# Attention at the head of a three-stage kernel: probabilities as the stationary operand, v moved, rows normalised per partition and then transposed

## The chip, the cores and the metric

One core of a Trainium2 chip runs the whole program. The metric is the device time in microseconds (us) of one execution; the kernel before has a median of 1134.29 us over three runs (1134.02 to 1134.41).

## What is computed

Three stages follow each other: attention over 4 batches of 8 heads (576 rows, head size 64), a feed-forward layer, and a layer of 8 experts. The change touches the first stage alone.

```python
scores = scale * np.matmul(q, k.transpose(0, 1, 3, 2))
thresh = np.max(scores, axis=-1, keepdims=True) - tau
scores = np.where(scores >= thresh, scores, -1000000000.0)
scores = scores - np.max(scores, axis=-1, keepdims=True)
attn = np.exp(scores)
attn = attn / (np.sum(attn, axis=-1, keepdims=True) + 1e-09)
return np.matmul(attn, v).astype(np.float32)
...
x = np.ascontiguousarray(attn_out.transpose(0, 2, 1, 3)).reshape(B * S, H * D)
x = _moe_ref(x=x, **moe_kwargs)
return _moe2_ref(x=x, **moe2_kwargs)
```

## The kernel before

Attention works on 16 pairs of heads. The 576 rows of a pair fall into five chunks, c = 0 to 4: four of 128 rows for each of the two heads, and a last one in which the 64 remaining rows of both heads share the 128 partitions. A step is one chunk of one pair, so a pair takes five steps, and the order of the work on each engine is written out by hand as a loop over steps (TensorE L435, ScalarE L514, VectorE L607, GpSimd L295).

What is done to one chunk is spread over several steps. In step c the chunk's scores lie in PSUM (`scores`, L339, issued at the end of the step before; three products of high and low halves of q and k in a shortened float format, both heads side by side in the array as 64-row tiles). VectorE copies them out with a running maximum (`maximum`, L560), GpSimd makes the exponent's bias and the cut from it, ScalarE takes the exponential (L477), and a step later VectorE masks and sums (`mask`, L570). Two steps later TensorE transposes the probabilities in sets of three blocks (`transposed_probs`, L358) into two PSUM banks `t_ps` in turn, ScalarE copies each set out to `probs_T` (`evacuate`, L480), and three steps later `output_main` (L376) multiplies with v. There v is the stationary operand, 64 columns of it, and the probabilities move: the even head writes partitions 0 to 63 of `o_ps`, the odd head partitions 64 to 127, so that two 64-column tiles of the array work side by side; one product with `v_mix`, 128 columns wide, takes the block that both heads share. The result is already transposed, which is how the next stage wants it (`x_T`).

The row sums lie along partitions, the result's rows along columns. So `broadcast_rinv` (L395) spreads the reciprocals with eight small products into `m_ps`, ScalarE copies them to `rinv_bc` (`copy_rinv`, L497), and VectorE multiplies (`normalise_main`, L586). `output_tail` (L410) does the same for the last chunk, with `copy_rinv_tail` and `normalise_tail`.

`m_ps` is one PSUM bank shared by turns. It also takes the transposes of the next pair's k, q and ends (`transposed_k` L307, `transposed_q` L316, `transposed_ends` L326), which ScalarE copies as high halves (`k_hi`, `q_hi`, `ends_hi`) and VectorE turns into low halves (`k_lo`, `q_lo`, `ends_lo`). A turn ends when the low half is done.

Two waits set the rhythm between TensorE and VectorE: scores of a step wait until both maxima of the step before are done (their two PSUM tiles are reused, L343), and the transposes of a chunk wait for its masks (L361). In a set's wait on `evac_done` (L363) the transposes wait for the set two before it to be copied out.

## Time and profile before

| | us |
|---|---|
| median of three runs | 1134.29 |
| lowest, highest | 1134.02, 1134.41 |
| the profiled execution: its time | 1132.23 |
| the profiled execution: its span, first to last instruction | 1130.5 |
| TensorE matmul busy, in all | 1046.8 (93% of the span) |
| weight loads busy | 925.7 (82%) |
| VectorE, ScalarE, GpSimd busy | 678.1, 556.1, 495.1 |
| mean granted TensorE clock | 0.977 |

Attention ends and the feed-forward layer's first product starts at 335.21 us of the span. In the trace an operand pair is written output<-moving,stationary or the other way round; which one is stationary is told by the weight load (PEld) rows. A product of 32-bit floats shows as two MATMUL records, each with its own weight load, called two passes here; a transpose shows as one. The form 128\*64 is a tile of 128 rows by 64 columns of the array, and what follows is the moving operand. Durations of matmuls overlap, so costs are read from one start to the next. c = 0 to 4 names the step; "two heads" marks scores of steps 0 to 3, "ends" those of step 4.

### The profile page before, as it was taken

The page shows a single profiled execution, that of the slowest core. Times are in us where ns is not written, and L with a number is a line of the kernel's source. Part 1 is how long each engine was busy: PE and PEld are TensorE (multiplying, and loading weights), DVE is VectorE, ACT ScalarE, POOL GpSimd, SP SyncE. Part 2 cuts the span into 40 slices and gives each one's busy share as a digit, 9 for nine tenths or more (in the row PEclk, how much of TensorE's full clock was granted, in tenths as well). Part 3 has the DMA queues.
Part 4 walks back from the last instruction along what each step waited for, and adds up shares of the span by engine and source line. Part 5 has one row for each costly group of instructions (what it writes and reads, how often), then busy time and mean ns, then how long its engine had stood idle before and what let it go on. Part 6 is the DMA issues. An engine that isn't in the chain of part 4 may idle for free. (4 is left out here: it accounts for less than half of the span.)

```text
span 1130.5 us, 22630 instructions
## 1 busy us (share of the span) xinstructions
PE 1046.8 (93%) x8153; PEld 925.7 (82%) x8153; DVE 678.1 (60%) x1336; ACT 556.1 (49%) x854; POOL 495.1 (44%) x734
## 2 busy tenths in 40 slices
PE   7999999999989999999899999997489999999995
PEld 5778787877769999999899989996377777777774
DVE  5887887878756534334334433433667777777773
ACT  4777777778753211211121112111367777777773
POOL 4777777777740000000000000000548888888973
PEclk9999999999999999999999999998599999999999
DMA  4323232232112100000000000002492573411100
GB/s 105 79 63 80 50 86 55 67 76 64 37 49 76 29 20 1 25 1 19 2 24 1 19 2 24 1 19 71 151 394 94 179 254 106 178 39 37 38 27 22
DMA packets 76314, 75.40 MB, mean 67 GB/s; under 512 B 48815, under 2 KB 54959, under 8 KB 76210
## 3 DMA queue, kind: packets, MB, share of 16 engines
q1 hardware_dynamic: 72690, 63.49, 18.4%
q0 software_dynamic: 3520, 10.49, 2.7%
q8 instruction: 69, 1.13, 0.4%
q14 instruction: 35, 0.29, 0.1%
HBM read 64.52 MB, written 10.49 MB: 66 GB/s over the span
## 5 line engine op out<-in xcount | busy, mean ns | idle before, releaser
L820 ACT ACTIVATE r_buf<-h_ps 128x288 f32<-128x288 f32 x128 | 52.6, 411 | 347.3 <-PE h_ps L777 347.3
L884 DVE TENSOR_TENSOR r_buf<-r_buf 128x288 f32<-128x288 f32 x128 | 58.7, 458 | 243.5 <-ACT r_buf L820 243.5
L1169 POOL MEMSET ones<- 128x128 bf16 x1 | 0.2, 209 | 453.0 <-POOLq L637 453.0
L1097 DVE TENSOR_TENSOR w_lo<-w_experts,w_hi 128x2048 fp32r<-128x2048 f32 x66 | 163.4, 2501 | 32.1 <-ACT w_hi L1336 32.1
L1336 ACT ACTIVATE w_hi<-w_experts 128x2048 fp32r x88 | 163.4, 1909 | 32.1 <-issue 14.0
L777 PE MATMUL h_ps<-x_hi,w_in_hi 128*128 128x288 f32 x512 | 154.4, 302 | 6.1 <-DVE x_lo L878 3.5
L777 PE MATMUL h_ps<-x_hi,w_in_lo 128*128 128x288 f32 x512 | 151.9, 297 | 3.1 <-issue 3.1
L777 PE MATMUL h_ps<-x_lo,w_in_hi 128*128 128x288 f32 x512 | 152.4, 298 | 0.0
L796 PE MATMUL y_ps<-g_hi,w_out_hi 128*128 128x288 f32 x512 | 151.4, 296 | 0.3 <-DVE g_lo L890 0.3
L796 PE MATMUL y_ps<-g_hi,w_out_lo 128*128 128x288 f32 x512 | 151.1, 295 | 0.0
L796 PE MATMUL y_ps<-g_lo,w_out_hi 128*128 128x288 f32 x512 | 151.0, 295 | 0.0
L477 ACT ACTIVATE e_sb<-s_sb,stats,live 128x576 f32<-128x576 f32 x144 | 124.4, 865 | 22.8 <-POOL stats L263 21.4
L576 DVE SCALAR_TENSOR_TENSOR probs<-s_sb,stats,e_sb 128x576 f32<-128x576 f32 x144 | 115.7, 835 | 1.5 <-POOL stats L276 1.4
L567 DVE TENSOR_SCALAR_CACHE_REDUCE s_sb<-s_ps 128x576 f32<-128x576 f32 x144 | 103.7, 754 | 19.0 <-PE s_ps L353 17.9
L777 PEld LDWEIGHTS h_ps<-x_hi,w_in_hi 128*128 128x128 f32 x512 | 97.2, 190 | 10.0 <-issue 9.9
L263 POOL TENSOR_SCALAR stats<-stats,minus_live 128x1 f32<-128x1 f32 x144 | 76.0, 528 | 61.3 <-DVE s_sb L567 60.8
L1097 POOL TENSOR_TENSOR w_lo<-w_experts,w_hi 128x2048 fp32r<-128x2048 f32 x22 | 101.9, 4633 | 2.0 <-ACT w_hi L1336 1.7
L495 ACT ACTIVATE probs_T<-t_ps 128x384 f32<-128x384 f32 x192 | 86.5, 485 | 32.6 <-PE t_ps L368 27.9
L777 PEld LDWEIGHTS h_ps<-x_hi,w_in_lo 128*128 128x128 f32 x512 | 97.6, 191 | 0.0
L777 PEld LDWEIGHTS h_ps<-x_lo,w_in_hi 128*128 128x128 f32 x512 | 97.4, 190 | 0.0
L796 PEld LDWEIGHTS y_ps<-g_hi,w_out_hi 128*128 128x128 f32 x512 | 96.6, 189 | 0.6 <-DVE g_lo L890 0.6
L796 PEld LDWEIGHTS y_ps<-g_hi,w_out_lo 128*128 128x128 f32 x512 | 96.6, 189 | 0.0
(196 smaller groups left out, 2407.0 us busy)
## 6 DMA issues: line engine op xcount, KB each, us to landing
w_experts<-in_moe_w_dram SPq DMA_DIRECT2D x16, 2048.0 KB, 13.9
k_raw<-in_k_dram SPq DMA_DIRECT2D x32, 128.0 KB, 3.1
q_raw<-in_q_dram SPq DMA_DIRECT2D x32, 128.0 KB, 3.0
w_raw<-in_moe_w_in_dram SPq DMA_DIRECT2D x16, 256.0 KB, 3.2
v_nat<-in_v_dram SPq DMA_DIRECT2D x16, 256.0 KB, 2.6
y_T<-in_moe_w_out_dram SPq DMA_DIRECT2D x16, 256.0 KB, 2.7
y_rows<-y_row SPq DMA_DIRECT2D x16, 256.0 KB, 2.2
v_odd<-in_v_dram SPq DMA_DIRECT2D x16, 64.0 KB, 2.3
```

The source lines that it names most:

```text
L263: V.tensor_scalar(stat(BIAS, step, h), stat(MAX, step, h), minus_live[:], None, ALU.mult).then_inc(bias_ready, 1)
L477: nc.scalar.activation(e_sb[step % 2][h][:], s_sb[step % 2][h][:], ACT.Exp, bias=stat(BIAS, step, h), scale=live[:]).then_inc(exp_done, 1)
L495: nc.scalar.activation(out, src[:], ACT.Copy).then_inc(evac_done, 1)
L567: V.tensor_scalar(halves(s_sb[step % 2][h][:]), s_ps[n % 2][:, :, 0:HALF], 1.0, None, ALU.mult, ALU.max, accum_out=stat(MAX, step, h)).the ...
L576: V.scalar_tensor_tensor(probs_of(c, h), s_sb[step % 2][h][:], stat(CUT, step, h), e_sb[step % 2][h][:], ALU.is_ge, ALU.mult, accum_out=su ...
L777: last = pe.matmul(h_ps[f % 2][:, 0:HALF], w, x[hf][:, kc, :], start=(kc == 0 and m == 0), stop=(kc == KC - 1 and m == 2))
L796: last = pe.matmul(y_ps[d][:, 0:HALF], w, g[f % 2][:], start=(f == 0 and m == 0), stop=(f == FC - 1 and m == 2))
L820: nc.scalar.activation(r_buf[f % 2][:], h_ps[f % 2][:, 0:HALF], ACT.Relu).then_inc(relu_done, 1)
L884: nc.vector.tensor_tensor(r[:], r[:], r[:], ALU.mult).then_inc(g_ops, 1)
L1097: alu.tensor_tensor(group_of(w_lo, g), raw_group(buf, g), group_of(w_hi, g).bitcast(F32), ALU.subtract).then_inc(done, 1)
L1169: nc.gpsimd.memset(ones[:], 1.0).then_inc(pool_set, 1)
L1336: nc.scalar.activation(group_of(w_hi, g), raw_group(buf, g), ACT.Copy).then_inc(hi_done, 1)
```

## The change

Seven things change, all in attention.

- `output_main`: the transposed probabilities become the stationary operand (128 columns), v moves (64 columns, and 128 for `v_mix`). The result has rows on partitions and is not transposed.
- `normalise_main` multiplies by the reciprocal per partition into a new tile `x_nat`; `broadcast_rinv`, `copy_rinv` and `copy_rinv_tail` are gone.
- `transposed_x` transposes `x_nat` with four transposes into `m_ps`, in step 3 of the next pair; ScalarE copies it to `x_T` (`copy_x`).
- `output_tail` moves from step 2 to step 3, waits for `copy_x`, and has five products 128 columns wide instead of twelve of 64; `normalise_tail` becomes two operations on 64 x 64 at the end of step 4; `transposed_x_tail` brings the two halves into place with one product against `ident2`, followed by a scores product in TensorE's order; ScalarE copies it in the step after.
- Ends are padded from 64 to 128 rows or columns with zeros (six more memsets in the set-up).
- Low halves move later on VectorE: `k_lo` from the end of step 0 to behind the maxima of step 1, `q_lo` from step 1 to the end of step 2, `ends_lo` from step 3 to behind the maximum of step 4. `q_hi` moves to step 2 and `ends_hi` to step 4 on ScalarE.
- `transposed_x` waits for `q_lo` of the next pair, `transposed_q` for `k_lo`.

```diff
@@ TensorE
             def output_main(i, c):
...
+                pt, even, odd = probs_T[m % 2], slice(c * P, c * P + D), slice(c * P + D, (c + 1) * P)
+                pe.matmul(o_ps[:, c * P:(c + 1) * P], pt[:, LAST, :], v_mix[b][:], start=True, stop=False,
+                          skip_group_check=True)
                 for kc in range(LAST):
-                    pe.matmul(o_ps[0:D, cols], v_nat[b][:, 0, kc, :], pt[:, kc, :],
-                              start=(c == 0 and kc == 0), stop=False, skip_group_check=True)
-                    pe.matmul(o_ps[D:P, cols], v_odd[b][:, kc, :], pt[:, LAST + 1 + kc, :],
-                              start=(c == 0 and kc == 0), stop=False, skip_group_check=True)
-                pe.matmul(o_ps[:, cols], v_mix[b][:], pt[:, LAST, :], start=False, stop=(c == LAST - 1),
-                          skip_group_check=True).then_inc(pv_done, 1)
+                    pe.matmul(o_ps[:, even], pt[:, kc, :], v_nat[b][:, 0, kc, :], start=False, stop=(kc == LAST - 1),
+                              skip_group_check=True)
+                for kc in range(LAST):
+                    last = pe.matmul(o_ps[:, odd], pt[:, LAST + 1 + kc, :], v_odd[b][:, kc, :], start=False,
+                                     stop=(kc == LAST - 1), skip_group_check=True)
+                last.then_inc(pv_done, 1)
...
             def output_tail(i):
                 b = i % 2
                 pe.wait_ge(evac_done, set_no(i, LAST, 1) + 1)
-                pe.wait_ge(rbc_done, i + 1)
+                pe.wait_ge(x_main_done, i + 1)
+                for kc in range(QC):
+                    last = pe.matmul(m_ps[:, TAIL_OUT:TAIL_OUT + P], tail_T[:, kc, :], v_nat[b][:, :, kc, :],
+                                     start=(kc == 0), stop=(kc == LAST))
+                last.then_inc(tail_set, 1)
+
+            def transposed_x(i):
+                pe.wait_ge(norm_done, i + 1)
                 if i + 2 < PAIRS:
                     pe.wait_ge(qlo_done, i + 3)
...
+                for c in range(LAST):
+                    last = pe.transpose(m_ps[:, c * P:(c + 1) * P], x_nat[:, c, :], ident[:])
+                last.then_inc(x_main_set, 1)
+
+            def transposed_x_tail(i):
+                pe.wait_ge(norm_tail_done, 2 * (i + 1))
...
+                pe.matmul(m_ps[:, TAIL_X:TAIL_X + TAIL], x_nat[:, LAST, :], ident2[:], start=True,
+                          stop=True).then_inc(x_tail_set, 1)
...
@@ VectorE
             def normalise_main(i):
                 dve.wait_ge(pv_done, LAST * (i + 1))
-                dve.wait_ge(rbc_done, i + 1)
-                V.tensor_tensor(x_T[:, i, 0:MAIN], o_ps[:], rinv_bc[:, 0:MAIN], ALU.mult).then_inc(x_main_done, 1)
+                dve.wait_ge(rinv_ready, i + 1)
+                if i >= 1:
+                    dve.wait_ge(x_main_set, i)
+                each = rinv[:, 0:2 * LAST].rearrange("p (n a) -> p n a", a=1).broadcast_to([P, 2 * LAST, D])
+                V.tensor_tensor(x_nat[:, 0:LAST, :].rearrange("p c (h d) -> p (c h) d", h=2),
+                                o_ps[:].rearrange("p (n d) -> p n d", d=D), each, ALU.mult).then_inc(norm_done, 1)
...
+                for h in range(2):
+                    rows = slice(h * TAIL, (h + 1) * TAIL)
+                    V.tensor_scalar(x_nat[rows, LAST, h * D:(h + 1) * D],
+                                    m_ps[rows, TAIL_OUT + h * D:TAIL_OUT + (h + 1) * D], rinv[rows, CHUNKS - 1:CHUNKS],
+                                    None, ALU.mult).then_inc(norm_tail_done, 1)
```

How the instructions stand now is shown for the two engines that wait for each other. First TensorE, from the transposes in step 2 on (L368 and L375 are the probabilities' transposes, L353 and L360 the scores). Before:

```order
L368 MATMUL t_ps<-ident,probs 128x128 x9
L417 MATMUL m_ps<-ident,rinv 64x64 x2
L423 MATMUL m_ps<-tail_T,v_nat 64x64 x10
L353 MATMUL s_ps<-kT_hi,qT_hi 128x288 x4
L353 MATMUL s_ps<-kT_lo,qT_hi 128x288 x4
L353 MATMUL s_ps<-kT_hi,qT_lo 128x288 x4
L368 MATMUL t_ps<-ident,probs 128x128 x6
```

The same place in the changed kernel, on through step 3:

```order
L375 MATMUL t_ps<-ident,probs 128x128 x9
L360 MATMUL s_ps<-kT_hi,qT_hi 128x288 x4
L360 MATMUL s_ps<-kT_lo,qT_hi 128x288 x4
L360 MATMUL s_ps<-kT_hi,qT_lo 128x288 x4
L375 MATMUL t_ps<-ident,probs 128x128 x6
L420 MATMUL m_ps<-ident,x_nat 128x128 x4
L394 MATMUL o_ps<-v_mix,probs_T 128x128
L397 MATMUL o_ps<-v_nat,probs_T 128x64 x4
L400 MATMUL o_ps<-v_odd,probs_T 128x64 x4
L375 MATMUL t_ps<-ident,probs 128x128 x3
L409 MATMUL m_ps<-v_nat,tail_T 128x128 x5
L343 MATMUL m_ps<-ident,q_raw 128x128
```

The tail's products have left step 2, which now holds nine transposes and the scores; they stand in step 3, together with the four new transposes of x.

Then VectorE, from the end of step 0 to step 3 (L567 and L570 are maxima, L576 and L579 masks, L543 and L546 `k_lo`, L548 and L551 `q_lo`, L589 and L595 `normalise_main`). Before:

```order
L543 TENSOR_TENSOR kT_lo<-m_ps,kT_hi 128x512
L584 RECIPROCAL rinv<-sums_eps 128x9
L567 TENSOR_SCALAR s_sb,stats<-s_ps 128x576 x2
L576 SCALAR_TENSOR_TENSOR probs,sums<-s_sb,stats,e_sb 128x576 x2
L548 SCALAR_TENSOR_TENSOR qT_lo<-m_ps,qT_hi 128x512
L567 TENSOR_SCALAR s_sb,stats<-s_ps 128x576 x2
L589 TENSOR_TENSOR x_T<-o_ps,rinv_bc 128x512
L576 SCALAR_TENSOR_TENSOR probs,sums<-s_sb,stats,e_sb 128x576 x2
L567 TENSOR_SCALAR s_sb,stats<-s_ps 128x576 x2
```

In the changed kernel:

```order
L570 TENSOR_SCALAR s_sb,stats<-s_ps 128x576 x2
L546 TENSOR_TENSOR kT_lo<-m_ps,kT_hi 128x512
L579 SCALAR_TENSOR_TENSOR probs,sums<-s_sb,stats,e_sb 128x576 x2
L587 RECIPROCAL rinv<-sums_eps 128x9
L570 TENSOR_SCALAR s_sb,stats<-s_ps 128x576 x2
L595 TENSOR_TENSOR x_nat<-o_ps,rinv 128x512
L579 SCALAR_TENSOR_TENSOR probs,sums<-s_sb,stats,e_sb 128x576 x2
L551 SCALAR_TENSOR_TENSOR qT_lo<-m_ps,qT_hi 128x512
L570 TENSOR_SCALAR s_sb,stats<-s_ps 128x576 x2
```

`q_lo` now stands behind the normalisation and both masks of step 2, where before it stood ahead of the maxima of that step.

## Rows read from the trace of the kernel before

**Rows 1.** The page, part 1: busy time by engine.

```profile
PE 1046.8 (93%) x8153; PEld 925.7 (82%) x8153; DVE 678.1 (60%) x1336; ACT 556.1 (49%) x854; POOL 495.1 (44%) x734
```

**Rows 2.** Stretches, one pair: us; busy PE, PEld, DVE, ACT, POOL; clock; DMA.

```profile
202.23:221.94 19.71, 19.24 (x219) 15.69 (x218) 15.93 (x44) 15.26 (x30) 14.68 (x39) 1.00 0.29 67
```

**Rows 3.** Timeline of TensorE, one pair: start, duration, then the instructions.

```profile
202.23 0.27 PE L336 MATMUL m_ps<-ident,q_raw 128*128 128x128 f32 x1
...
202.63 0.53 PE L353 MATMUL s_ps<-kT_hi,qT_hi 128*128 128x288 f32 x2
...
204.28 0.32 PE L388 MATMUL o_ps<-probs_T,v_nat 128*64 128x128 f32 x1
...
205.63 0.49 PE L368 MATMUL t_ps<-ident,probs 128*128 128x128 f32 x3
206.05 0.53 PE L353 MATMUL s_ps<-kT_hi,qT_hi 64*128 64x288 f32 x4
...
210.04 0.54 PE L353 MATMUL s_ps<-kT_hi,qT_hi 64*128 64x288 f32 x4
...
211.23 1.09 PE L405 MATMUL m_ps<-ident,rinv 128*64 128x128 f32 x16
212.26 0.66 PE L371 MATMUL t_ps<-ident,probs 128*128 128x128 f32 x4
...
215.82 0.88 PE L368 MATMUL t_ps<-ident,probs 128*128 128x128 f32 x6
217.04 0.52 PE L368 MATMUL t_ps<-ident,probs 128*128 128x128 f32 x3 [0.34 <-ACT probs_T L495]
217.49 0.33 PE L417 MATMUL m_ps<-ident,rinv 128*64 128x64 f32 x4
217.65 0.90 PE L423 MATMUL m_ps<-tail_T,v_nat 128*64 128x64 f32 x20
218.48 0.53 PE L353 MATMUL s_ps<-kT_hi,qT_hi 64*128 64x288 f32 x4
...
219.46 0.87 PE L368 MATMUL t_ps<-ident,probs 128*128 128x128 f32 x6
```

**Rows 4.** Timelines of TensorE and its weight loads, second stage: 128 stationary columns.

```profile
401.38 0.60 PE L749 MATMUL row_ps<-ident,y_T 128*128 128x128 f32 x4
401.81 0.96 PE L751 MATMUL logit_ps<-gates,y_T 128*128 128x16 f32 x8
401.70 0.97 PEld L751 LDWEIGHTS logit_ps<-gates,y_T 128*128 128x128 f32 x8
402.59 0.19 PEld L777 LDWEIGHTS h_ps<-x_hi,w_in_hi 128*128 128x128 f32 x1
```

**Rows 5.** Timeline of VectorE in the same pair.

```profile
215.57 0.69 DVE L548 SCALAR_TENSOR_TENSOR qT_lo<-m_ps,qT_hi 128x512 fp32r<-128x512 f32 x1 [1.51 <-ACT qT_hi L466]
...
217.53 0.69 DVE L589 TENSOR_TENSOR x_T<-o_ps,rinv_bc 128x512 f32<-128x512 f32 x1
218.13 0.81 DVE L576 SCALAR_TENSOR_TENSOR probs<-s_sb,stats,e_sb 128x576 f32<-128x576 f32 x1
...
218.86 0.82 DVE L576 SCALAR_TENSOR_TENSOR probs<-s_sb,stats,e_sb 128x576 f32<-128x576 f32 x1
...
219.60 0.76 DVE L567 TENSOR_SCALAR_CACHE_REDUCE s_sb<-s_ps 128x576 f32<-128x576 f32 x1
...
220.28 0.76 DVE L567 TENSOR_SCALAR_CACHE_REDUCE s_sb<-s_ps 128x576 f32<-128x576 f32 x1
```

**Rows 6.** Groups by line, 50 to 320 us: busy, mean ns, idle before.

```profile
L501 ACT ACTIVATE rinv_bc<-m_ps 128x512 f32<-128x512 f32 x14 | 8.4, 597 | 14.1 <-PE m_ps L405 14.1
...
L593 DVE TENSOR_TENSOR x_T<-m_ps,rinv_bc 128x64 f32<-128x64 f32 x14 | 3.1, 221 | 0.0
```

**Rows 7.** Timeline of TensorE at the end of attention.

```profile
330.20 0.49 PE L392 MATMUL o_ps<-probs_T,v_mix 128*128 128x128 f32 x2
...
335.21 0.58 PE L777 MATMUL h_ps<-x_hi,w_in_hi 128*128 128x288 f32 x1 [3.53 <-DVE x_lo L878]
```

More of the change, by code:

```diff
@@ L134, in attention @@
         rinv = sb("rinv", [P, CHUNKS])
-        rinv_bc = sb("rinv_bc", [P, S])
+        x_nat = sb("x_nat", [P, QC, P])
+        ident2 = sb("ident2", [P, TAIL])
         tau_col = sb("tau_col", [P, 1])
@@ L178, in attention @@
         WPIECE = WPART // LAST
+        SETUP = 14
+        Q_END, K_END, TAIL_OUT, TAIL_X = 0, P, 2 * P, 3 * P
         def qk_bank(i, kind):
@@ L372, in transposed_probs @@
                 else:
-                    last = pe.transpose(out[0:TAIL, 0:P], probs[c][:, MAIN:S], ident[:])
+                    last = pe.transpose(out[:, 0:P], probs[c][:, S - P:S], ident[:])
                 last.then_inc(probs_set, 1)
@@ L392, in output_main @@
-                pe.matmul(o_ps[:, cols], v_mix[b][:], pt[:, LAST, :], start=False, stop=(c == LAST - 1),
-                          skip_group_check=True).then_inc(pv_done, 1)
-            def broadcast_rinv(i):
-                pe.wait_ge(rinv_ready, i + 1)
-                if i + 2 < PAIRS:
-                    pe.wait_ge(klo_done, i + 3)
-                else:
-                    pe.wait_ge(elo_done, 2 * PAIRS)
-                    pe.wait_ge(x_tail_done, i)
-                    pe.wait_ge(rbc_tail_done, i)
-                for c in range(LAST):
-                    for par in range(2):
-                        last = pe.matmul(m_ps[D * par:D * (par + 1), c * P:(c + 1) * P],
-                                         rinv[:, 2 * c + par:2 * c + par + 1].broadcast_to([P, D]), ident[:],
-                                         start=True, stop=True)
-                last.then_inc(rinv_set, 1)
+                    pe.matmul(o_ps[:, even], pt[:, kc, :], v_nat[b][:, 0, kc, :], start=False, stop=(kc == LAST - 1),
+                              skip_group_check=True)
@@ L434, in _ @@
             scores(0, 0)
-            for step in range(STEPS * PAIRS + 3):
+            for step in range(STEPS * PAIRS + STEPS):
                 i, c = divmod(step, STEPS)
                 made, used = divmod(step - 2, STEPS), divmod(step - 3, STEPS)
-                if c == 1 and i >= 1:
-                    broadcast_rinv(i - 1)
                 if 0 <= made[0] < PAIRS:
@@ L444, in _ @@
                     transposed_k(i + 1)
-                if 0 <= used[0] and used[1] < LAST:
+                if c == 3 and i >= 1:
+                    transposed_x(i - 1)
+                if 0 <= used[0] < PAIRS and used[1] < LAST:
                     output_main(*used)
@@ L450, in _ @@
                     transposed_q(i + 1)
-                if 0 <= used[0] and used[1] == LAST:
-                    output_tail(used[0])
+                if c == 3 and i >= 1:
+                    output_tail(i - 1)
                 if c == 3 and i + 1 < PAIRS:
                     transposed_ends(i + 1)
+                if c == 4 and i >= 1:
+                    transposed_x_tail(i - 1)
                 if step + 1 < STEPS * PAIRS:
@@ L513, in _ @@
             act.wait_ge(live_set, 2)
-            for step in range(STEPS * PAIRS + 3):
+            for step in range(STEPS * PAIRS + STEPS + 1):
                 i, c = divmod(step, STEPS)
                 made = divmod(step - 2, STEPS)
-                if c == 1 and i >= 1:
-                    copy_rinv(i - 1)
+                if c == 0 and i >= 2:
+                    copy_x_tail(i - 2)
+                if c == 4 and i + 1 < PAIRS:
+                    ends_hi(i + 1)
                 if 0 <= made[0] < PAIRS:
@@ L525, in _ @@
                     k_hi(i + 1)
+                if c == 2 and i + 1 < PAIRS:
+                    q_hi(i + 1)
+                if c == 3 and 1 <= i <= PAIRS:
+                    copy_x(i - 1)
                 if 0 <= made[0] < PAIRS and sets_in(made[1]) == 3:
                     evacuate(*made, 2)
[L528 to L533 removed]
                 if i < PAIRS and len(heads_in(c)) == 2:
@@ L606, in _ @@
             ends_lo(0)
-            for step in range(STEPS * PAIRS + 4):
+            for step in range(STEPS * PAIRS + STEPS):
                 i, c = divmod(step, STEPS)
@@ L612, in _ @@
                         maximum(i, c, h)
+                if c == 1 and i + 1 < PAIRS:
+                    k_lo(i + 1)
                 if c == 2 and i >= 1:
                     normalise_main(i - 1)
-                if c == 3 and i >= 1:
-                    normalise_tail(i - 1)
+                if c == 4 and i + 1 < PAIRS:
+                    ends_lo(i + 1)
                 if 0 <= before[0] < PAIRS:
@@ L619, in _ @@
                         mask(*before, h)
-                if c == 0 and i + 1 < PAIRS:
-                    k_lo(i + 1)
-                if c == 0 and i >= 1:
+                if c == 1 and i >= 1:
                     reciprocal(i - 1)
-                if c == 1 and i + 1 < PAIRS:
+                if c == 2 and i + 1 < PAIRS:
                     q_lo(i + 1)
-                if c == 3 and i + 1 < PAIRS:
-                    ends_lo(i + 1)
+                if c == 4 and i >= 1:
+                    normalise_tail(i - 1)
 EARLY = HALF // P
```

97 lines of the change are left out of this document (45 added, 52 removed).

## The prediction

> **What bounds the kernel now.** I began with the busy shares: TensorE is busy for 93% of the span, no other engine for more than 60% [rows 1]. Then I cut out one pair of attention: from one transpose of the ends to the same one of the next pair is 19.71 us, with TensorE busy for 19.24, VectorE 15.93, ScalarE 15.26, at full clock (1.00, the 2.4 GHz level) [rows 2]. The two pairs after it read the same. So attention is TensorE's queue, read start to start. It stands still in two places: nine transposes in step 2 take from 215.82 to 217.04 before the last three begin, because both banks wait for ScalarE's copy, where six in a row would take 0.71; that is 0.51. And from scores to the broadcast of the reciprocals is 1.19 (210.04 to 211.23), from scores to transposes 0.98 (218.48 to 219.46), so 0.21 there. Waits are 0.7 a pair, work is 19.0 [rows 3]. Whatever TensorE gets more of is paid in full.
>
> **Prices.** Four transposes take 0.43 (401.38 to 401.81), so 0.108 each [rows 4]. Three transposes and a change of the array's tile shape take 0.42 (205.63 to 206.05): a change costs 0.10 [rows 3]. The form that decides is a float product with 128 stationary columns and few moving: its eight passes have eight weight loads, from 401.70 to the next load at 402.59, 0.111 each [rows 4]. These passes move only 16 columns, so moving less doesn't help: the load sets the pace. The other bound is what a pass costs if its 64 moving columns decide: the tail's 20 passes in side-by-side pairs need 0.83 (217.65 to 218.48); less two changes of shape that is 0.063 a pair [rows 3]. I take 0.111, since its row has the same stationary width; the tail's has half of it.
>
> **The multiplication with v.** Before: 204.28 to 205.63 is 1.35, plus the change into 64-column tiles 0.10, so 1.45 [rows 3]. Now nine products of two passes, 18 x 0.111 = 2.00, and no change of shape. That is +0.55 a chunk, +2.2 a pair. The eight pairs of passes that ran side by side at 0.109 (0.87 together) become 16 in a row (1.78), and only two changes of shape come off. The Trainium skill, TensorEngine Tiling (Array Packing), When to Use Tiling, recommends the opposite swap where the moving side has 64 columns or fewer: make it stationary and use two column tiles, up to twice as fast. By that rule 0.87 becomes 1.74, and the trace agrees with it. Its Key Properties say that a change of tiling mode drains the engine, which speaks for the change; the trace prices that at 0.10.
>
> **The rest of TensorE's work, per pair** [rows 3].
> - Broadcasts go: 211.23 to 212.26, -1.03.
> - The tail: 217.49 to 218.48 is 0.99; now 5 x 2 passes at 0.111 = 1.11; +0.12.
> - Four transposes of x: +0.43. Joining the tail's halves: 2 passes, +0.22.
> - Ends: 202.23 to 202.63 is 0.40; now two full transposes without a change of shape, 0.22; -0.18.
> - The last probability block, 128 columns for 64: same slot, 0.
> Sum: 2.2 - 1.03 + 0.12 + 0.43 + 0.22 - 0.18 = +1.8 a pair; work becomes 20.8.
>
> **The waits.** Time 0 is here the start of the scores of chunk 2, which TensorE issues at the end of step 1. VectorE's first maximum starts 1.12 later (218.48 to 219.60), each takes 0.68 (219.60 to 220.28), the normalisation 0.60 (217.53 to 218.13), a mask 0.73 (218.13 to 218.86), and a result is seen by TensorE at its full duration plus about 0.06, a mask's and a maximum's with 0.08 more for the accumulator [rows 5]. In the changed order VectorE does: maxima at 1.12 and 1.80, normalisation at 2.49, masks at 3.09 and 3.83, `q_lo` at 4.57 (done 5.32), maxima of step 3 at 5.18 and 5.86, masks to 8.0.
> - Step 2 on TensorE: transposes at 0.98, the last three at 2.20 behind ScalarE as before, scores at 2.65. The maxima allow 2.63. Without the tail nothing else fills this step. Wait 0.51.
> - Step 3: transposes could begin at 3.63; the first mask is seen at 3.93 (wait 0.30), the second at 4.67 (0.36), `q_lo` at 5.32 (0.30). Then transposes of x, v (2.00), three transposes: 8.12. The tail needs `copy_x` on ScalarE, which stands behind an exponential fed by the maximum at 5.18; I put its end at 7.8, 0.60 long [rows 6], so just in time. Tail and ends: scores of chunk 4 at 9.45.
> - Step 4: VectorE has the maximum at 10.54, `ends_lo`, two masks, then the two halves of the tail's normalisation, each at most the 0.22 of today's [rows 6], and done near 13.5. TensorE would be there at 13.3. Wait 0.15, scores at 13.8. Behind `transposed_x_tail` stand the next pair's first scores, so this wait would be everybody's.
> - Step 0 takes 4.55; step 1 4.12, and `k_lo` is seen 3.24 after its scores where TensorE needs it at 3.59: no wait.
> Waits are 1.67 and the period 13.8 + 4.55 + 4.12 = 22.47 against 19.71: +2.77. VectorE (about 16 busy) and ScalarE keep up over the whole pair; it is their order in steps 2 and 3 that binds. GpSimd is at 14.68 of 19.71 [rows 2] and keeps pace in each step but the shortest, where it has slack till the masks.
>
> **The ends of the stage.** Fourteen full pairs: +38.8. The first has two chunks only, +0.9. The last one waits more for its masks in any case and loses k, q and ends in both kernels, +2.2. Then a chain that was short before: from the last product with v (330.20) to the next stage's first (335.21) is 5.0 [rows 7]. New in line are the normalisation 0.69, transposes 0.43 and copy 0.60, and the tail, its normalisation, joining and copy follow one after another: about 3.6 of work for 1.4, and four more hand-overs of 0.2 (a transpose runs 0.27, its slot is 0.11 [rows 3]); +3.2. More memsets and `ident2` at the start hide behind the first loads; without that cover they would be 1.5. Loads of v start a step later and still have most of a pair. Sum: 38.8 + 0.9 + 2.2 + 3.2 = **+45**. The profiled execution was 1132.23, its span 1130.5; it becomes 1177. The median is 2.1 above it, so 1179.
>
> **Rivals.**
> - *The order absorbs its waits.* VectorE and ScalarE run ahead in the long steps, waits stay at 0.7. For it: `q_lo` has 1.51 of idle time ahead of it today [rows 5]. Against it: the maxima of chunk 2 can't start before its scores. +1.8 x 16 + 3 = +32, less for the ends of the stage, 1165.
> - *More waits than I traced.* `copy_x` comes late behind the exponential, or the tail's normalisation does: each delay passes through to the scores. One more us a pair gives +61, 1195.
> - *Loads hide in part.* A pass half-way between the bounds, 0.087: v 1.57 a chunk, but then `copy_x` holds step 3 and VectorE step 4; traced again the period is 21.1, +1.4 x 15 + 3 = +24, 1158. The Trainium skill, TensorE: Matmul & The Clock Gate, Back-to-back issue gap, gives about 81 ns a matmul for load-and-multiply streams of 128; the estimate by it is 1156. Rows 4 speak against it here.
> - *Faster.* A pass costs what its 64 moving columns cost, 0.063. The 84 passes a pair save 4.0, work is 16.8. With waits as today the period is 17.5, or -2.2 x 15 + 3 = -30, 1104; it decides from a pass below 0.090 (the 1.8 of more work over 84). Against it: the 16-column passes, and by my trace VectorE's order would still hold the period at 20.4 (1147).
> - *No change.* It would need a pass near 0.090 and waits that don't grow; nothing in the rows gives both.
> A clock that falls is no rival: the single waits are under 0.6 and clock stayed at 1.00 over such waits [rows 2].
>
> **How the numbers follow.** Forecast 0.58; waits absorbed 0.15; more waits 0.15; loads hidden in part 0.06; faster 0.03; no change 0.02; more than all of these 0.01. The range takes in the forecast, the absorbed waits and half of the third, and a pass at 0.108 or 0.114 (4 us): 1163 to 1193, leaving out 0.06 + 0.07 + 0.06, about 0.2. A measurement of this kernel can tell 0.2%, 2.3 us. Faster 0.03, same 0.02, slower 0.95.
>
> **What would show it.** The period of a pair near 22.5. The passes of the product with v 0.11 apart, a chunk 2.0. TensorE idle in step 2 before the last three transposes, and in step 3 ahead of both sets and ahead of the transposes of x, released by VectorE's masks and `q_lo`; almost no wait at the tail. No records at 64-column tiles in attention. The second stage's first product near 380. I am wrong if passes of `output_main` are closer than 0.09, if the period is under 21.4 or over 23.5, or if waits stand mostly elsewhere, for instance at `transposed_x_tail`.

## The result and the profile after

The changed kernel takes 1184.81 us (median of four runs, 1183.98 to 1186.32) against 1134.15 for the kernel before (four runs, 1132.51 to 1134.41): a ratio of 1.0451, with a 95% interval of 1.0433 to 1.0469. That is 50.7 us more. The profiled execution of the changed kernel took 1186.32 with a span of 1184.6, so the spans differ by 54.1.

The busy shares, part 1 of the page of the changed kernel, answer to [rows 1]:

```profile
PE 1085.9 (92%) x7769; PEld 986.3 (83%) x7769; DVE 679.3 (57%) x1359; ACT 555.9 (47%) x854; POOL 489.2 (41%) x734
```

TensorE has fewer records than before (7769 for 8153) and is busy for 39 us longer; the others do what they did. One pair, in the view of stretches, answers to [rows 2]:

```profile
207.25:229.82 22.57, 21.45 (x196) 19.26 (x195) 15.92 (x44) 15.18 (x30) 14.52 (x39) 1.00 0.24 60
```

The period is 22.57 for 19.71. The 54.1 us of span fall into four pieces, read at the last scores, at the first product of the second stage and at the first of the third:

| | before | after | difference |
|---|---|---|---|
| last scores of attention | 319.96 | 363.92 | +44.0 |
| from there to the second stage's first product | 15.25 | 19.05 | +3.8 |
| second stage (code unchanged) | 453.6 | 458.8 | +5.2 |
| third stage (code unchanged) | 341.7 | 342.8 | +1.1 |

The rows that they are read at, besides the two first products of the second stage (335.21 and 382.97): before,

```profile
319.96 0.51 PE L353 MATMUL s_ps<-kT_hi,qT_hi 128*128 128x288 f32 x2
...
788.82 0.31 PE L1220 MATMUL he_ps<-ohb,earlier 128*128 128x160 bf16 x1 [4.78 <-DVE ohb L1397]
```

and changed,

```profile
363.92 0.51 PE L360 MATMUL s_ps<-kT_hi,qT_hi 128*128 128x288 f32 x2
...
841.76 0.32 PE L1238 MATMUL he_ps<-ohb,earlier 128*128 128x160 bf16 x1 [4.78 <-DVE ohb L1415]
```

The timeline of TensorE in that pair answers to [rows 3] (start, duration, instructions):

```profile
208.93 0.39 PE L394 MATMUL o_ps<-v_mix,probs_T 128*128 128x128 f32 x2
209.15 1.00 PE L397 MATMUL o_ps<-v_nat,probs_T 128*128 128x64 f32 x8
209.99 1.06 PE L400 MATMUL o_ps<-v_odd,probs_T 128*128 128x64 f32 x8
210.89 0.50 PE L375 MATMUL t_ps<-ident,probs 128*128 128x128 f32 x3
211.62 0.43 PE L428 MATMUL m_ps<-ident,x_nat 128*128 128x64 f32 x2 [0.23 <-DVE x_nat L604]
211.98 0.53 PE L360 MATMUL s_ps<-kT_hi,qT_hi 64*128 64x288 f32 x4
...
220.58 0.53 PE L360 MATMUL s_ps<-kT_hi,qT_hi 64*128 64x288 f32 x4
...
222.79 0.52 PE L375 MATMUL t_ps<-ident,probs 128*128 128x128 f32 x3 [0.34 <-ACT probs_T L502]
223.24 0.54 PE L360 MATMUL s_ps<-kT_hi,qT_hi 64*128 64x288 f32 x4
...
224.51 0.55 PE L375 MATMUL t_ps<-ident,probs 128*128 128x128 f32 x3 [0.20 <-DVE probs L579]
225.25 0.55 PE L375 MATMUL t_ps<-ident,probs 128*128 128x128 f32 x3 [0.19 <-DVE probs L579]
225.95 0.63 PE L420 MATMUL m_ps<-ident,x_nat 128*128 128x128 f32 x4
...
228.70 1.28 PE L409 MATMUL m_ps<-v_nat,tail_T 128*128 128x128 f32 x10
229.82 0.27 PE L343 MATMUL m_ps<-ident,q_raw 128*128 128x128 f32 x1
```

Two things are to be seen. Eight passes of L397 take 0.84 (209.15 to 209.99), so 0.105 each, and a whole chunk takes 2.0 (208.93 to 210.89). And between 223.24 and 225.95 both sets of transposes stand behind VectorE's masks. VectorE's own timeline shows why (it answers to [rows 5]):

```profile
221.68 0.76 DVE L570 TENSOR_SCALAR_CACHE_REDUCE s_sb<-s_ps 128x576 f32<-128x576 f32 x1 [0.44 <-PE s_ps L360]
...
223.03 0.69 DVE L595 TENSOR_TENSOR x_nat<-o_ps,rinv 128x512 f32<-128x512 f32 x1
223.64 0.81 DVE L579 SCALAR_TENSOR_TENSOR probs<-s_sb,stats,e_sb 128x576 f32<-128x576 f32 x1
...
224.37 0.81 DVE L579 SCALAR_TENSOR_TENSOR probs<-s_sb,stats,e_sb 128x576 f32<-128x576 f32 x1
...
225.11 0.69 DVE L551 SCALAR_TENSOR_TENSOR qT_lo<-m_ps,qT_hi 128x512 fp32r<-128x512 f32 x1
...
231.04 0.76 DVE L570 TENSOR_SCALAR_CACHE_REDUCE s_sb<-s_ps 128x576 f32<-128x576 f32 x1 [2.41 <-PE s_ps L360]
```

The maximum of chunk 2 can't start before its scores (220.58), and from 221.68 to 225.71 VectorE has no gap; the transposes of x wait for `q_lo` at the end of it. Once the masks of step 3 are done, VectorE is idle for 2.41, and TensorE is the late one. Each engine waits for the other within one pair.

### The profile page after: what moved, and what is told of

Its sections match the earlier page's. It is cut to its first block and busy times, and to the rows that moved or that the text cites. A ratio compares the mean times of both kernels' runs of the same rounds, so it can differ in the third digit from the quotient of the medians.

```text
span 1184.6 us, 21885 instructions
## 1 busy us (share of the span) xinstructions
PE 1085.9 (92%) x7769; PEld 986.3 (83%) x7769; DVE 679.3 (57%) x1359; ACT 555.9 (47%) x854; POOL 489.2 (41%) x734
## 5 line engine op out<-in xcount | busy, mean ns | idle before, releaser
L570 DVE TENSOR_SCALAR_CACHE_REDUCE s_sb<-s_ps 128x576 f32<-128x576 f32 x144 | 103.9, 755 | 104.6 <-PE s_ps L360 104.6
L502 ACT ACTIVATE probs_T<-t_ps 128x384 f32<-128x384 f32 x192 | 89.3, 491 | 98.3 <-PE t_ps L375 97.3
L579 DVE SCALAR_TENSOR_TENSOR probs<-s_sb,stats,e_sb 128x576 f32<-128x576 f32 x144 | 112.4, 813 | 1.1 <-POOL stats L283 0.6
L270 POOL TENSOR_SCALAR stats<-stats,minus_live 128x1 f32<-128x1 f32 x144 | 61.2, 425 | 107.0 <-DVE s_sb L570 106.7
L375 PE MATMUL t_ps<-ident,probs 128*128 128x128 f32 x576 | 91.5, 281 | 11.4 <-DVE probs L579 6.0
## 6 DMA issues: line engine op xcount, KB each, us to landing
w_experts<-in_moe_w_dram SPq DMA_DIRECT2D x16, 2048.0 KB, 13.4
```

The costliest lines, as they stand in the source:

```text
L270: V.tensor_scalar(stat(BIAS, step, h), stat(MAX, step, h), minus_live[:], None, ALU.mult).then_inc(bias_ready, 1)
L375: last = pe.transpose(out[:, j * P:(j + 1) * P], probs[c][:, blk * P:(blk + 1) * P], ident[:])
L502: nc.scalar.activation(out, src[:], ACT.Copy).then_inc(evac_done, 1)
L570: V.tensor_scalar(halves(s_sb[step % 2][h][:]), s_ps[n % 2][:, :, 0:HALF], 1.0, None, ALU.mult, ALU.max, accum_out=stat(MAX, step, h)).the ...
L579: V.scalar_tensor_tensor(probs_of(c, h), s_sb[step % 2][h][:], stat(CUT, step, h), e_sb[step % 2][h][:], ALU.is_ge, ALU.mult, accum_out=su ...
```

## Experiments

Theory A is the prediction's: the weight loads set the pace of the new passes, and VectorE's order adds the waits. The rivals stand with each expectation. Every kernel is compared with the kernel before in runs of the same session, of 1133.2 to 1134.7 us. "Period" is that of a pair, "attention" the time of the second stage's first product (before 335.21, changed 382.97).

**1. Without the odd head's products.** This kernel leaves out four of the nine products of each chunk, so half the result is missing; the experts then get other rows, and its time in the third stage (328.5 for 342.8) means nothing here.

```diff
-                for kc in range(LAST):
-                    last = pe.matmul(o_ps[:, odd], pt[:, LAST + 1 + kc, :], v_odd[b][:, kc, :], start=False,
...
```

> The changed kernel without the four products of the odd head in the multiplication with v (8 of 18 passes a chunk are left out, so half of the attention's result is not computed). Theory A (TensorE bound in steps 0 and 1, bound by the other engines' order in steps 3 and 4): step 0 loses 0.89 us; step 1 only 0.34, since k_lo is seen 3.2 after its scores; step 3 only 0.27, since copy_x ends 7.7 after the scores of chunk 2; step 4 nothing, since the tail's normalisation is what it waits for. The pair gets shorter by 1.5, 22.57 to 21.1, the time by 21 to 24 us against the changed kernel, about 1161 to 1164. Theory B (TensorE's work alone sets the period): 4 x 0.89 = 3.55 us a pair, 22.57 to 19.0, about 1130.

Measured: attention 362.05 (-20.9), period 21.20 (-1.37); ratio in all 1.0147 (1.0123 to 1.0171). TensorE in one chunk, and at the joining:

```profile
200.18 0.43 PE L425 MATMUL m_ps<-ident,x_nat 128*128 128x64 f32 x2 [1.12 <-DVE x_nat L601]
...
202.69 0.39 PE L394 MATMUL o_ps<-v_mix,probs_T 128*128 128x128 f32 x2
202.91 1.00 PE L397 MATMUL o_ps<-v_nat,probs_T 128*128 128x64 f32 x8
203.75 0.50 PE L375 MATMUL t_ps<-ident,probs 128*128 128x128 f32 x3
```

The chunk takes 1.06 (202.69 to 203.75) for 2.0, so the eight missing passes were worth 0.9, 3.6 a pair, but the period falls by 1.37 only: the joining (`transposed_x_tail`, here L425) now stands 1.12 for the tail's normalisation, and in the other steps other waits grow. Steps 0, 1, 3 and 4 lose 0.89, 0.24, 0.23 and 0.01, where theory A had 0.89, 0.34, 0.27 and 0; theory B's period of 19.0 is out. Both halves of theory A show: the price of a pass, and a VectorE that would hold the period near 21 with far less work on TensorE. It also shows that work and waits can't simply be added.

**2. Low halves back in their old places** on VectorE and ScalarE, the rest as in the changed kernel.

```diff
-                if c == 1 and i + 1 < PAIRS:
-                    k_lo(i + 1)
...
+                if c == 0 and i + 1 < PAIRS:
+                    k_lo(i + 1)
...
-                if c == 2 and i + 1 < PAIRS:
+                if c == 1 and i + 1 < PAIRS:
                     q_lo(i + 1)
+                if c == 3 and i + 1 < PAIRS:
+                    ends_lo(i + 1)
```

> The changed kernel with the low halves and the high halves of q and of the ends back in the places they had before the change. Theory A (what is late in step 3 is the last of a chain on VectorE, and moving q_lo ahead only shifts the maxima of chunk 2 by as much as it frees later): steps 2 and 3 stay within 0.1 us, step 4 loses 0.3 because ends_lo leaves it, and the first pair's stand of 2.7 goes: 4 to 8 us less than the changed kernel, 1177 to 1181. Theory B (the later low halves are what makes the new order work): the maxima of chunk 2 come late with nothing gained, 0.3 to 0.5 us more a pair, 1189 to 1193.

Measured: 1176.90, ratio 1.0382 (1.0356 to 1.0408), period 22.14, attention 375.08. So the moved low halves are a loss by themselves, 7.9 of the 50.7 us: 0.43 in each period, and two more in the first pair. Of the 0.43, step 4 gives 0.34 and step 3 0.27, and step 2 takes back 0.17; theory A had steps 2 and 3 unchanged. That first-pair stand is this row of the changed kernel:

```profile
18.23 1.09 PE L333 MATMUL m_ps<-ident,q_raw 128*128 128x128 f32 x4 [2.23 <-DVE kT_lo L546]
```

`transposed_q` waits 2.23 for `k_lo`, which in the first pair stands behind maxima that come late. With `k_lo` in step 0 this is gone, and the scores of the second pair start at 29.39 instead of 31.46.

**3. The tail's normalisation ahead of the masks** in step 4.

```diff
+                if c == 4 and i >= 1:
+                    normalise_tail(i - 1)
                 if 0 <= before[0] < PAIRS:
...
                     q_lo(i + 1)
-                if c == 4 and i >= 1:
-                    normalise_tail(i - 1)
```

> The changed kernel with the tail's normalisation ahead of the two masks in VectorE's step 4 instead of behind them. Theory A: TensorE no longer waits before it joins the tail's halves; the wait of 0.3 us a pair goes, 4 to 5 us in all, 1180; the masks come 0.3 later and are still early for step 0. Theory B (the wait is covered by the scores' own wait for maxima): no difference, 1184 to 1185.

Measured: 1178.62, ratio 1.0392 (1.0366 to 1.0418), period 22.07; step 4 is 4.08 instead of 4.59. The joining no longer stands:

```profile
207.29 0.50 PE L375 MATMUL t_ps<-ident,probs 128*128 128x128 f32 x3
207.63 0.33 PE L428 MATMUL m_ps<-ident,x_nat 128*128 128x64 f32 x2
207.89 0.53 PE L360 MATMUL s_ps<-kT_hi,qT_hi 64*128 64x288 f32 x4
```

It starts 0.34 after the three transposes, for 0.73 in the changed kernel (210.89 to 211.62), and the scores follow it by 0.26 for 0.36 (211.62 to 211.98). So the wait cost 0.39, and starting from a stand 0.10 more. It was one on the path of everything, as the prediction said, and bigger than the 0.15 that the prediction gave and the 0.3 of the expectation.

**4. Two column tiles.** Each product keeps the probabilities stationary, but in two halves of 64 columns, side by side; v moves. It computes the same.

```diff
                 for kc in range(LAST):
-                    pe.matmul(o_ps[:, even], pt[:, kc, :], v_nat[b][:, 0, kc, :], start=False, stop=(kc == LAST - 1),
-                              skip_group_check=True)
+                    for half in (slice(0, D), slice(D, P)):
+                        pe.matmul(o_ps[half, even], pt[:, kc, half], v_nat[b][:, 0, kc, :], start=False,
+                                  stop=(kc == LAST - 1), skip_group_check=True)
...
```

> The changed kernel with each product of v_nat and v_odd split into two 64-column tiles side by side (the two halves of the stationary probabilities), so the layout of the result stays transposed to what it was but no load is 128 columns wide there. Theory A (the load of 128 columns sets the pace of a pass): a pair of passes takes 0.058 as in the tail before, a chunk 0.93 + 0.22 + two changes of shape 0.2 = 1.35 against 2.0; steps 0, 1, 3, 4 lose 0.65, 0.34, 0.27, 0: 1.3 us a pair, 22.57 to 21.3, about 1165. Theory B (a pass costs about 0.11 whatever its width, and two tiles from one stationary tile don't run side by side): 32 passes in a row, a chunk of 3.5 or more, 1270 or worse.

Measured: 1169.35, ratio 1.0314 (1.0288 to 1.0341), period 21.59. TensorE in one chunk:

```profile
208.88 0.39 PE L394 MATMUL o_ps<-v_mix,probs_T 128*128 128x128 f32 x2
209.19 0.69 PE L398 MATMUL o_ps<-v_nat,probs_T 128*64 128x64 f32 x16
209.71 0.64 PE L402 MATMUL o_ps<-v_odd,probs_T 128*64 128x64 f32 x16
210.57 0.63 PE L333 MATMUL m_ps<-ident,q_raw 128*128 128x128 f32 x4 [0.23 <-DVE kT_lo L548]
```

Sixteen passes in eight pairs take 0.52 (209.19 to 209.71), where eight full passes took 0.84; the chunk is 1.46 (208.88 to 210.34, which is 210.57 less the 0.23 of idle) for 2.0, both changes of shape included. A pair of passes with 64 stationary columns each takes 0.065 where one with 128 takes 0.105, and the moving side is 64 columns in both: it is the stationary side that sets the pace. 15 us of the loss come back.

For 64 moving columns the Trainium skill, TensorEngine Tiling (Array Packing), When to Use Tiling, recommends to swap the operands and use two column tiles; that is not this kernel, in which v still moves, but the product of the kernel before. The trace agrees with the page so far as that product takes 1.45 a chunk and the changed kernel's untiled one 2.0. Tiles without the swap come out level with it, at 1.46.

More than half of the saving, 1.2 of 4 x 0.54 = 2.2 a pair, is again lost to waits, since the period falls by 0.98 only (theory A had 1.3). The list of waits from 50 to 315 us (total, times, longest) names TensorE's largest:

```profile
PE m_ps L430 <- DVE x_nat L606: 9.6, 13, 0.7
```

**5. The kernel before, with k's ends padded**, to see what one kept idea of the change is worth alone.

```diff
-                pe.transpose(bank[:, P:P + TAIL], k_raw[b][0:TAIL, LAST, :], ident[0:TAIL, 0:TAIL]).then_inc(ends_set, 1)
+                pe.transpose(bank[:, P:2 * P], k_raw[b][:, LAST, :], ident[:]).then_inc(ends_set, 1)
...
+                V.memset(k_raw[b][TAIL:P, LAST, :], 0.0).then_inc(setup_done, 1)
```

> The kernel before with one part of the change alone: the ends of k padded with zeros to 128 rows, so that their transpose needs no change of the array's shape. Theory A (a change of shape is on TensorE's path and costs 0.1): 0.40 becomes 0.22 once a pair, 0.18 x 15 = 2.7 us less, 1131.6. Theory B (the time is absorbed by the wait for the masks behind it): no difference over 0.5 us.

Measured: 1131.07, ratio 0.9984 (0.9968 to 1.0000), too near to 1 to call a gain; the period of 19.70 speaks for theory B. Step 3 falls from 3.87 to 3.60, and step 0 takes it back (3.99 to 4.47, with step 1 down by 0.20). The list of waits names what is late next; before, this line read 12.0 in total and at most 0.7:

```profile
ACT e_sb L477 <- POOL stats L263: 21.8, 26, 1.5
```

**6. The kernel before, with the tail between the transposes' sets** in step 2, where TensorE stands for ScalarE's copy [rows 3].

```diff
+                if 0 <= used[0] and used[1] == LAST:
+                    output_tail(used[0])
                 if 0 <= made[0] < PAIRS and sets_in(made[1]) == 3:
...
-                if 0 <= used[0] and used[1] == LAST:
-                    output_tail(used[0])
```

> The kernel before with the tail's products of step 2 placed between the second and the third set of transposes, where TensorE stands 0.5 us for ScalarE's copy. Theory A (the next wait takes most of it: the masks of step 2 are seen 4.1 and 4.9 us after its scores, and step 3 now wants them at 4.2 and 4.6): step 2 shorter by 0.4, step 3 longer by 0.25, 2 to 3 us less in all, 1132. Theory B (the wait simply goes): 6 us less, 1128.

Measured: 1133.45, ratio 0.9995 (0.9981 to 1.0009), period 19.68. Step 2 falls from 3.65 to 3.26 and step 3 grows from 3.87 to 4.21. The wait was filled, and the masks of step 2 became the wait, as in theory A: before their transposes the weight loads now stand for VectorE's `probs` 26 times, 6.7 us in all from 50 to 315, in a line that the kernel before doesn't have.

**7. The kernel before, with both and two more moves**: the broadcast of the reciprocals behind the transposes, and `normalise_main` behind the masks of step 2.

```diff
-                if c == 1 and i >= 1:
-                    broadcast_rinv(i - 1)
                 if 0 <= made[0] < PAIRS:
                     for s in range(2):
                         transposed_probs(*made, s)
+                if c == 1 and i >= 1:
+                    broadcast_rinv(i - 1)
...
```

> The kernel before with padded ends, the tail between the sets, the broadcast of the reciprocals behind the transposes of step 1 instead of ahead of them, and the normalisation behind the masks of step 2, so that they come 0.6 earlier. Theory A: the pair loses 0.18 + 0.4 + 0.2, with the masks no longer late; 0.7 to 0.8 us a pair, 10 to 12 us in all, 1122 to 1124. Theory B (a new wait, at the multiplication that needs the normalised bank free, takes half): 5 us less, 1129.

Measured: 1129.55, ratio 0.9967 (0.9952 to 0.9981), period 19.43: -0.28 where 0.7 to 0.8 was forecast. Steps 2 and 3 kept their gains (3.27, 3.61), but step 0 is 4.71 for 3.99:

```profile
204.50 0.52 PE L368 MATMUL t_ps<-ident,probs 128*128 128x128 f32 x3 [0.51 <-ACT probs_T L495]
```

The list of waits of this kernel has `ACT e_sb L477 <- POOL stats L263` at 28.5 us. TensorE waits for a copy, ScalarE's copy stands behind an exponential, and that for GpSimd's bias, on the least busy of the four engines; GpSimd in turn waits for VectorE's maxima (39.1 us in all). By the trace this chain is the next bound of the kernel before; no run tests it. The time is theory B's 1129, but the wait is not the one that B named: at the multiplication with v the list has no wait of TensorE for the normalisation. The forecast had left the chain through GpSimd out.

**8. Column tiles and VectorE's order mended.** Experiments 2, 3 and 4 together, `normalise_main` behind the masks of step 2, and `copy_x` ahead of the exponential in step 3.

```diff
...
                         mask(*before, h)
+                if c == 2 and i >= 1:
+                    normalise_main(i - 1)
+                if c == 0 and i + 1 < PAIRS:
+                    k_lo(i + 1)
...
+                if c == 3 and 1 <= i <= PAIRS:
+                    copy_x(i - 1)
                 if i < PAIRS:
                     exponential(i, c, 0)
...
```

> The changed kernel with column tiles in the multiplication with v, the tail's normalisation ahead of the masks of step 4, low halves in their old places, the normalisation behind the masks of step 2, and the copy of x ahead of the exponential in step 3. Theory A (with short passes the rest of the loss is waits that an order can take away): steps 0 to 4 at 4.0, 3.6, 2.8, 5.9 and 3.6, the pair 19.9 against 19.71 before; with 4 us more at the end of attention and the 5 us more that the second stage takes in all kernels of this form so far, 1144 to 1148. Theory B (the extra hand-overs of the transposed result keep step 3 long whatever the order): the pair at 20.7 or more, 1156 or above.

Measured: 1138.28, ratio 1.0034 (1.0022 to 1.0047), attention 335.74. That is 6 us below theory A's range; steps 4, 0, 1 and 2 are as it had them, and step 3 takes 5.62 for 5.9. One pair, in the view of stretches:

```profile
213.32:232.93 19.61, 19.10 (x260) 16.42 (x259) 16.07 (x45) 15.32 (x29) 14.54 (x39) 1.00 0.29 70
```

Here TensorE's work (19.10) and the period (19.61) are those of the kernel before, to 0.15. All that the change cost in attention is therefore in two things, the form of the product with v and the order of the other engines' work. How the loss divides between them is not shown: alone, experiments 4, 2 and 3 give back 15.5, 7.9 and 6.2 us, all together with two more moves 46.5, and no run has the whole new order with full passes. This kernel is still 4 us slower than before, with its attention over at the same time (335.74 for 335.21): its second stage takes 458.7, for 453.6. The changed kernel and its forms so far (experiments 1 to 4 and 8) all take 458.3 to 460.2 there, the kernel before and its forms 452.0 to 454.9, though none touches that stage.

**9 and 10. The same kernels with the second stage's code further on.** TensorE's warm-up at the start has eight transposes of `ident`; here it has 24, each with its weight load, and nothing else is changed. They run beside the first loads.

```diff
-                for c in range(LAST):
+                for c in tuple(range(LAST)) * 3:
                     pe.transpose(t_ps[bank][:, c * P:(c + 1) * P], ident[:], ident[:])
```

> The changed kernel with 16 more warm-up transposes at its start, in time in which TensorE waits for the first loads. They move all later instructions of TensorE by 32 places and cost nothing by themselves. In five kernels of the changed form the second stage, whose code is the same, took 458.3 to 460.2 us from its first product to the third stage's, against 453.6 before: at its two returns to the loop's start TensorE stands 2.7 to 3.2 us instead of 1.7 to 2.0, and runs at the 1.2 GHz level for 6.8 us after each. Theory A (the place of the loop's code among the instructions decides how long the return takes): the second stage's time moves by over 1.5 us. Theory B (it is something else, such as the size of the program or what the other engines do): it stays at 458 to 460.

> The kernel before with the same 16 more warm-up transposes. Theory A (place of the loop's code): the second stage moves away from 453.6 by over 1.5 us. Theory B: it stays within 1 us of it, and the whole within 1 us of the kernel before.

Measured: the changed kernel 1174.35, ratio 1.0360 (1.0343 to 1.0377); the kernel before 1125.29, ratio 0.9925 (0.9909 to 0.9942). Periods are as they were (22.57, 19.71), the second stages 445.3 both. So 8 to 13 us of that stage hang on how many instructions stand ahead of it. The difference of the two kernels is now 49.1 us, nearly all of it in attention (first products at 383.08 and 334.81, 48.3). So with the code placed alike the change costs nothing in the second stage.

The traces show the mechanism. First TensorE in the changed kernel, where its loop over batches returns to its start:

```profile
598.73 0.39 PE L795 MATMUL h_ps<-x_hi,w_in_hi 128*128 128x288 f32 x1 [1.82 <-issue]
601.46 0.61 PE L795 MATMUL h_ps<-x_lo,w_in_hi 128*128 128x288 f32 x1 [2.33 <-issue]
```

It stands twice, for nothing that the profile shows. The list of TensorE's waits over the stage has four such stands, 7.9 us in all:

```profile
PE h_ps L795 <- issue: 7.9, 4, 2.3
```

That is 4.2 and 3.8 at the two returns. In the kernel before it is 5.6 in all, 3.0 and 2.7 (the expectation's 2.7 to 3.2 for 1.7 to 2.0 is not what the rows show), and in experiments 9 and 10 the line is missing. The granted clock is the third column from the end in the stretches:

```profile
597.00:610.00 13.00, 8.94 (x50) 8.73 (x51) 3.22 (x9) 1.53 (x4) 0.00 (x0) 0.74 0.01 3
550.00:597.00 47.00, 46.91 (x357) 46.67 (x356) 18.34 (x43) 7.79 (x17) 0.00 (x0) 1.00 0.04 13
```

After a stretch at 2.4 GHz without a gap the engine stood 1.82 and 2.33 us, and a mean of 0.74 means that about half of the 13 us were at 1.2 GHz; from 712 to 725, at the second return, it is 0.74 again. In the kernel before the clock stays at 1.00 from 556 to 569, behind the first return, and is 0.88 from 665.6 to 678.6, behind the second. The whole stage, of the kernel before and of the changed kernel:

```profile
335.20:788.80 453.60, 440.54 (x3312) 437.97 (x3312) 184.61 (x439) 84.22 (x187) 1.13 (x7) 0.98 0.07 21
383.00:841.70 458.70, 443.38 (x3312) 440.59 (x3312) 184.74 (x439) 84.22 (x187) 1.13 (x7) 0.97 0.07 20
```

and of experiment 9:

```profile
383.10:828.40 445.30, 437.89 (x3312) 435.98 (x3312) 184.51 (x439) 84.10 (x187) 1.14 (x7) 0.99 0.06 20
```

The same 3312 records are busy for 5.5 us more in the changed kernel than in experiment 9, at the lower mean clock; with the 7.9 of stands that is the 13.4 between the two. Of the 5.2 between the two kernels 2.3 are stands and 2.8 are busy time. Then the queue of instructions in the DMA view. The changed kernel over the later passes of the loop, 610 to 838 us:

```profile
q8 instruction: 16, 0.26, 0.5%
```

and the same code in experiment 9, 600 to 820 us:

```profile
q8 instruction: 1, 0.02, 0.0%
```

Over the whole stage it is 32 packets of 16 KB for 14. Where the loop's instructions lie badly, every pass loads them again, and at the return TensorE waits for them; where they lie well, one pass loads them and the later ones bring nothing.

The queue does not say for which engine a packet is; that these are TensorE's is read from the stands, beside which they arrive (three packets from 594 to 604 us, and no other traffic) and with which they go. The kernel before has 31 packets and shorter stands, so the packets alone don't give the price of a return.

The Trainium skill, Runtime: NRT & Kernel Launch, Instruction fetch mechanics, says that TensorE has room for 2048 instructions, refilled in blocks of 16 KB or 256 instructions, and that a taken branch whose target isn't in the current two-page window makes it stand for the transfer. The trace agrees in the size of the packets and in the stands, but not in the two pages: in experiment 9 a pass of the loop, 828 matmul records and as many weight loads, is run again without a stand. The page's 2048 would fit that, and also explain why the boundary is so near (1656 instructions and more may touch one block more or less), but that part is argued, not shown.

**11 and 12. The same shift on experiments 8 and 7.**

> The reordered kernel with column tiles (1138.3 us, a pair 19.61, second stage 458.7) with the 16 more warm-up transposes. Theory A (place of the loop's code; both forms of attention have then the same second stage): the second stage falls to 445.3 as in both kernels that had them, 13 us less, 1125, level with the kernel before plus the same transposes (1125.3). Theory B (the gain came from where the two tried kernels happened to land, and this one lands elsewhere): the second stage stays near 458 or takes any value between.

> The reordered kernel of the old form (1129.6 us, second stage 452.0) with the 16 more warm-up transposes. Theory A: the second stage falls to 445.3, 6 to 7 us less, 1122 to 1123, the fastest of all. Theory B: it stays near 452.

Measured: column tiles in the mended order 1126.20, ratio 0.9929 (0.9914 to 0.9944); the kernel before in the order of experiment 7 1119.94, ratio 0.9880 (0.9861 to 0.9899). Second stages are 445.6 and 445.7. The first equals experiment 10 (0.9925): with the code placed alike, probabilities stationary is worth nothing, even if everything else is done for it. The second beats both kernels, by 13.2 us the one before: 8.4 from the place of the code, some 5 from the order.

## Why the prediction was right, and where it was off

The forecast was slower with 0.95, 1179 in 1163 to 1193; measured was 1184.8. Step by step:

- **TensorE's queue bounds attention.** Right: it is busy for 21.45 of the 22.57, at a granted clock of 1.00.
- **A pass costs 0.111, its load's pace.** Right in kind, 5% too high: 0.105 within a run of eight, 0.112 with the step to the next group (209.99 to 210.89 is eight passes). The chunk came to the 2.0 forecast. The 0.063 of the moving columns is out. The about 81 ns a matmul of the Trainium skill, TensorE: Matmul & The Clock Gate, Back-to-back issue gap, is not borne out either: the nearest row here is the 0.105.
- **The trace of waits.** Counted from the scores of chunk 2 (220.58), forecast and measured: last three transposes 2.20 and 2.21; scores 2.65 and 2.66; first mask seen 3.93 and 3.93; second 4.67 and 4.67; transposes of x 5.32 and 5.37; tail 8.12 and 8.12; scores of chunk 4 at 9.45 and 9.38. This is what tracing two engines against each other can do, where the sum of TensorE's work alone would have given 1.8 for a true 2.86 a pair. `copy_x` was just in time as forecast, ready at 7.7:

```profile
226.91 0.87 ACT L484 ACTIVATE e_sb<-s_sb,stats,live 128x576 f32<-128x576 f32 x1 [0.58 <-POOL stats L270]
227.68 0.58 ACT L506 ACTIVATE x_T<-m_ps 128x512 f32<-128x512 f32 x1
```

- **The wait at the joining, 0.15.** Too small: it is 0.39, and 0.10 more for starting from a stand (experiment 3), so step 4 takes 4.59 for the 4.35 forecast. Steps 0, 1 and 3 came out 0.03, 0.04 and 0.08 short, so the period is 22.57 for 22.47; that it is so near is in part luck, since errors of both signs cancel. The waits that the prediction lists make 1.62, not the 1.67 that it takes; nothing hangs on it.
- **The start and the first pair, +0.9.** The longer set-up hides, as forecast: the first scores start at 10.88 for 10.89. The pair was mis-sized: +2.6 (the ends' transposes at 27.41 for 24.81), or +2.3 at the scores behind them, where 0.26 of padding has come off. The step "the first has two chunks only" priced its products and not its order; `k_lo` behind the maxima cost 2.23 there, and experiment 2 removes it.
- **Fourteen full pairs, +38.8, and the last one, +2.2.** Measured from scores to scores +39.3 and +2.35.
- **The closing chain, +3.2.** Measured +3.8 from the last scores; from the last product with v, where the prediction starts it (330.20, changed about 373.9), +4.1. Its own terms add up to 3.0. Its length was right in kind; it ran with TensorE mostly standing, at a granted clock of 0.71 from 373 to 383 us, for 0.90 in the kernel before from 330 to 335.2:

```profile
375.10 0.66 PE L420 MATMUL m_ps<-ident,x_nat 128*128 128x128 f32 x4 [0.79 <-DVE x_nat L595]
376.53 1.80 PE L409 MATMUL m_ps<-v_nat,tail_T 128*128 128x128 f32 x10 [0.78 <-ACT x_T L506]
379.03 0.69 PE L428 MATMUL m_ps<-ident,x_nat 128*128 128x64 f32 x2 [0.69 <-DVE x_nat L604]
382.97 0.58 PE L795 MATMUL h_ps<-x_hi,w_in_hi 128*128 128x288 f32 x1 [3.25 <-DVE x_lo L896]
```

  The ten passes of the tail take 1.80 here and 1.28 in a full pair. Against "a clock that falls is no rival": within attention that held; at its end and in the second stage it did not.
- **Attention in all, +45.** Measured +47.8. What the sum had no term for is the second stage, +5.2: I took unchanged code to take unchanged time. In span the forecast is 9.1 short: 2.8 in attention, 5.2 in the second stage and 1.1 in the third. That the median is only 5.8 off is luck: it rose 3.4 less than the span of the profiled execution.
- **The rivals.** Waits were not absorbed. The second rival named two places. `copy_x` holds the tail in no full pair, only in the closing chain (0.78 at 376.53). The tail's normalisation does come late, by 0.24 a pair more in step 4 than forecast, a quarter of the 1 us that the rival priced. Experiment 1 tests the trace of VectorE: taking 3.6 of work off TensorE leaves a period of 21.20. The fast rival's period with VectorE as the bound was put at 20.4 for less work still; that number was not tested.

## What to carry to other kernels

Before turning an operand round, price the pass and not the columns: with 128 stationary columns a pass of 32-bit floats took 0.105 to 0.112 us whether 16, 64 or 128 columns moved, so a swap that leaves 64 moving must be split into column tiles to get even. Then write down both engines' order and trace one period; each gap that is filled uncovers the next wait (a mask, a copy, GpSimd's bias), and that one sets the gain. When a kernel has a long loop, look at the instruction queue in its DMA view before believing any difference below one per cent in another stage.

## What the hardware showed that I had not expected

Sixteen more transposes at the start, 0.1 to 0.2 us each, made the whole program 8.4 to 10.5 us faster, since they moved the loop of the second stage: 445.3 instead of 453.6 and 458.8, with 14 instruction packets for 31 and 32. And in the changed kernel the stands at a return cost twice, once as stands (7.9 us) and once by the granted clock behind them (5.5 us of busy time); the list of waits names only the first.
